# Regrouped attention products and re-placed loads in a fused gated-attention and feed-forward kernel

## The reference

```python
f = 1.0 / (1.0 + np.exp(-f_logit))            # q, k, v, f_logit: 4 x 8 x 768 x 48
for t in range(S):
    state = f[:, :, t, :, None] * state + einsum('bhd,bhe->bhde', k[:, :, t], v[:, :, t])
    y[:, :, t] = einsum('bhd,bhde->bhe', q[:, :, t], state)
x = y as (3072 tokens, 384)
h = x @ w_in;  x = where(h > 0, h, exp(min(h, 0)) - 1) @ w_out       # 384 -> 2048 -> 384
h = x @ w_in2; out = (maximum(h, 0) ** 2) @ w_out2                   # 384 -> 2048 -> 384
```

## Time and profile before

| | |
|---|---|
| median of 3 runs | 978.47 us (978.26 to 981.43) |
| profiled execution | 977.67 us |
| its span | 975.9 us, 27520 instructions |
| busy | PE 953.0 us (98%), PE's weight loads 786.8 (81%), DVE 504.7 (52%), ACT 402.1 (41%), POOL 237.8 (24%) |
| mean granted clock of TensorE | 0.996 |
| DMA | 56.87 MB, mean 58 GB/s |

### The profile page before, as it was taken

How to read it: one execution, slowest core, us unless ns; L and a number is a source line. 1 busy time by engine, 2 the same in 40 slices (tenths; PEclk the granted TensorE clock), 3 DMA queues, 4 the chain that set the end, 5 groups by cost and what they waited for, 6 DMA issues and landing times.

```text
span 975.9 us, 27520 instructions
## 1 busy us (share of the span) xinstructions
PE 953.0 (98%) x11636; PEld 786.8 (81%) x11636; DVE 504.7 (52%) x746; ACT 402.1 (41%) x706; POOL 237.8 (24%) x193
## 2 busy tenths in 40 slices
PE   7799989999999999999999999999999999999998
PEld 6677777888888788888878888888888888888897
DVE  7788576565757657563326663343343343433432
ACT  4555545344535443454444453242332422423322
POOL 3002215363635464454423641000000000000000
PEclk9999999999999999999999999999999999999999
DMA  7461422303130212212003331002020020020100
GB/s 240 152 195 41 127 67 68 99 2 100 36 97 24 79 65 69 65 48 68 1 2 109 97 86 66 1 8 58 1 50 14 0 61 3 7 57 0 19 15 33
DMA packets 72426, 56.87 MB, mean 58 GB/s; under 512 B 37248, under 2 KB 64640, under 8 KB 72320
## 3 DMA queue, kind: packets, MB, share of 16 engines
q1 hardware_dynamic: 69472, 43.87, 16.7%
q10 hardware_dynamic: 2848, 11.44, 3.3%
HBM read 45.84 MB, written 9.44 MB: 57 GB/s over the span
## 4 chain that ended last, share of the span: by engine, by line
PE 94%; DVE 2%; issue 2%; ACT 1%; DMA 1%; SPq 0%; DVEq 0%; ACTq 0%
PE ps L1669 8%; PE ps L1665 8%; PE ps L1664 8%; PE ps L1139 7%; PE ps L1688 7%; PE ps L1684 7%; PE ps L1685 7%; PE ps L1278 6%; PE ps L1301 6%; PE ps L1280 5%; PE ps L1287 5%; PE ps L1303 5%; PE ps L1307 5%; PE ps L1208 2%; PE ps L1156 1%
## 5 line engine op out<-in xcount | busy, mean ns | idle before, releaser
L1609 DVE TENSOR_TENSOR g<-g 128x512 f32<-128x512 f32 x96 | 66.8, 696 | 240.9 <-ACT g L1524 240.3
L1524 ACT ACTIVATE g<-ps 128x512 f32<-128x512 f32 x112 | 67.0, 598 | 276.9 <-PE ps L1669 272.6
L694 POOL TENSOR_TENSOR glo<-g,ghi 128x512 fp32r<-128x512 f32 x65 | 89.7, 1379 | 194.0 <-ACT ghi L519 194.0
L1664 PE MATMUL ps<-xhi,wts 128*128 128x512 f32 x336 | 130.9, 390 | 0.0
L1665 PE MATMUL ps<-xhi,wts 128*128 128x512 f32 x336 | 130.9, 390 | 0.0
L878 DVE SCALAR_TENSOR_TENSOR g<-e,g 128x512 f32<-128x512 f32 x80 | 57.9, 724 | 140.3 <-ACT g L513 140.3
L512 ACT ACTIVATE e<-ps 128x512 f32<-128x512 f32 x80 | 47.9, 598 | 162.6 <-PE ps L1287 162.6
L1684 PE MATMUL ps<-ghi,wts 128*128 128x512 f32 x294 | 114.4, 389 | 0.0
L1685 PE MATMUL ps<-ghi,wts 128*128 128x512 f32 x294 | 114.4, 389 | 0.0
L1278 PE MATMUL ps<-xhi,wts 128*128 128x512 f32 x240 | 98.9, 412 | 0.2 <-ACT g L513 0.2
L1669 PE MATMUL ps<-xlo,wts 128*128 128x512 f32 x336 | 94.6, 390 | 0.0
(11 more groups left out here) (132 smaller groups left out, 1559.4 us busy)
## 6 DMA issues: line engine op xcount, KB each, us to landing
raw<-w SPq DMA_DIRECT2D x52, 192.0 KB, 2.4
q<-qk SPq DMA_DIRECT2D x22, 256.0 KB, 5.0
gate<-fl SPq DMA_DIRECT2D x10, 512.0 KB, 5.5
k<-qk SPq DMA_DIRECT2D x10, 512.0 KB, 3.7
x<-xo ACTq DMA_DIRECT2D x6, 768.0 KB, 3.3
xs<-x ACTq DMA_DIRECT2D x6, 768.0 KB, 4.4
v<-vn SPq DMA_DIRECT2D x11, 384.0 KB, 4.0
krow<-vn SPq DMA_DIRECT2D x20, 192.0 KB, 4.5
```

Source lines behind the costliest of these rows:

```text
L694: nc.gpsimd.tensor_tensor(out=glo[:, f % 2, :], in0=g[:, f % 2, :], in1=ghi[:, f % 2, :].bitcast(F32), op=ALU.subtract).then_inc(s_glo, 1)
L1664: nc.tensor.matmul(h, w(0, k), xhi[:, k, :], start=(k == 0), stop=False)
```

## The change

The steady period of PE has five groups of small products: `product(c, h, 4)` (with `last_column` of the unit before in front of it, from unit 5 on), 5 and 0, 6 and 1, 2 and the transposes, and one of 288: q_state part 0, product 3 of the next unit, q_state part 1, both values and new_state. Slot 15 of a unit moves behind the first group of the next. The last unit keeps six groups. PSUM banks of level 2 change from unit 5 on (`level_pair`), and with them PE's waits. SP, ACT, POOL and DVE are reordered to match; `acc_copy` becomes three copies with a semaphore each. In the start and in the first two periods SP's loads move, DVE's takes of level 1 come before the activation that preceded them, and weight splits move later. The diff, cut to its core:

```diff
...
+        if past(c, h, 5):
+            return pair(c, h, "Y" if l < 2 else "A")
         if past(c, h, 3):
...
         return 2 * c + h + n < UNITS
+
+    def unit_before(c, h):
+
+        return divmod(2 * c + h - 1, 2)
...
         def period(c, h):
-            f = 8 * h
             if more(c, h, 2):
                 load_gates(c, h + 2)
-            if more(c, h, 2):
                 load_k(c, h + 2)
+                load_q(c, h + 2)
             if more(c, h):
+                sp.wait_ge(*level(s_mm, c, h + 1, 4))
                 load_v(c, h + 1)
                 load_staged_v(c, h + 1)
-            if more(c, h, 2):
-                load_q(c, h + 2)
...
             sp.wait_ge(*level(s_mm, 1, 0, 1))
+            load_weights(range(18, 20))
+            load_gates(1, 2)
+            sp.wait_ge(*level(s_mm, 1, 0, 2))
             load_staged_v(1, 0)
-            load_weights(range(18, 20))
-            sp.wait_ge(*level(s_mm, 1, 0, 2))
+            load_weights(range(20, 22))
+            sp.wait_ge(*level(s_mm, 1, 0, 4))
+            load_weights(range(22, 24))
             load_v(1, 0)
-            load_weights(range(20, 22))
-            sp.wait_ge(*level(s_mm, 1, 0, 3))
-            load_gates(1, 2)
-            load_weights(range(22, 24))
             sp.wait_ge(*level(s_mm, 1, 1, 1))
...
             load_k(1, 3)
+            load_q(1, 3)
+            sp.wait_ge(*level(s_mm, 1, 2, 4))
             load_v(1, 2)
             load_staged_v(1, 2)
-            load_q(1, 3)
...
         sp.wait_ge(*level(s_mm, 0, 0, 1))
-        load_weights(range(0, 2))
+        load_gates(1, 1)
+        load_weights(range(1))
         sp.wait_ge(*level(s_mm, 0, 0, 2))
+        load_q(1, 0)
+        sp.wait_ge(*level(s_mm, 0, 1, 1))
+        load_weights(range(1, 2))
         load_staged_v(0, 0)
-        load_gates(1, 1)
-        sp.wait_ge(*level(s_mm, 0, 0, 3))
-        load_weights(range(2, 4))
-        sp.wait_ge(*level(s_mm, 0, 1, 2))
-        load_weights(range(4, 6))
         sp.wait_ge(*level(s_mm, 0, 0, 4))
         load_staged_v(0, 1)
-        load_weights(range(6, 7))
-        sp.wait_ge(*level(s_mm, 0, 1, 3))
-        load_weights(range(7, 9))
+        load_v(0, 0)
         sp.wait_ge(*level(s_mm, 0, 0, 5))
-        load_weights(range(9, 10))
-        load_v(0, 0)
-        sp.wait_ge(*level(s_mm, 0, 1, 4))
-        load_weights(range(10, STAGED))
-        sp.wait_ge(*level(s_mm, 0, 1, 5))
+        load_weights(range(2, 4))
+        sp.wait_ge(*level(s_mm, 0, 0, 6))
         load_v(0, 1)
-        load_q(1, 0)
-        sp.wait_ge(s_kT, 1)
         load_k(1, 0)
+        load_weights(range(4, 6))
+        sp.wait_ge(s_y, 1)
+        load_weights(range(6, STAGED))
         sp.wait_ge(s_last, 1)
...
                 act.wait_ge(s_x2, c * 16 - 32)
-            nc.scalar.activation(xo[:, :, :], ps[:, ACC:ACC + KD, :], ACT.Copy).then_inc(s_acc, 1)
+            for m in range(KD):
+                done = nc.scalar.activation(xo[:, m, :], ps[:, ACC + m, :], ACT.Copy)
+                done.then_inc(s_acc if m == KD - 1 else s_accs, 1)
...
             f = 8 * h
+            if past(c, h, 5):
+                y_copy(*unit_before(c, h))
             hidden_copies(c, f - 1)
...
             hidden_copies(c, f)
+            take5(c, h)
+            high(c, f)
             if h == 0:
                 acc_copy(c)
-            high(c, f)
             hidden_copies(c, f + 1)
-            take5(c, h)
             if h == 0:
...
             high(c, f + 1)
+            pad_v(c, h)
+            take6(c, h)
             hidden_copies(c, f + 2)
             high(c, f + 2)
-            pad_v(c, h)
-            take6(c, h)
             hidden_copies(c, f + 3)
...
             high(c, f + 5)
-            y_copy(c, h)
             hidden_copies(c, f + 6)
+            if not more(c, h):
+                y_copy(c, h)
             high(c, f + 6)
...
         gates(1, 0, True)
-        split_weights(range(0, 2))
         gates(1, 1, True)
+        split_weights(range(0, 1))
         nc.scalar.activation(warm[:, 1:2], warm[:, 0:1], ACT.Exp)
+        split_weights(range(1, 2))
         pad_v(0, 0)
-        split_weights(range(2, 3))
         take4(0, 0)
-        split_weights(range(3, 4))
         take5(0, 0)
...
         take5(0, 1)
+        split_weights(range(2, 4))
         take6(0, 1)
...
             f = 8 * h
+            k_update(c, h, 4)
             low(c, f - 1)
-            k_update(c, h, 4)
             if more(c, h):
                 keep_last(c, h + 1)
+            k_update(c, h, 5)
+            low(c, f)
+            if more(c, h):
                 k_update(c, h + 1, 0)
-            low(c, f)
-            k_update(c, h, 5)
+            low(c, f + 1)
+            k_update(c, h, 6)
             if more(c, h):
                 k_update(c, h + 1, 1)
-            low(c, f + 1)
             low(c, f + 2)
-            k_update(c, h, 6)
+            low(c, f + 3)
             if more(c, h):
                 k_update(c, h + 1, 2)
-            low(c, f + 3)
+            low(c, f + 4)
             if more(c, h):
                 k_update(c, h + 1, 3)
-            low(c, f + 4)
             decay_state(c, h)
...
             f = 8 * h
+            step(c, h, 4)
             activate(c, f - 1)
...
                 x_split(c)
-            if more(c, h):
-                take(c, h + 1, 0)
-            q_update(c, h, 4)
-            take(c, h, 4)
-            if more(c, h):
-                q_update(c, h + 1, 0)
-                double(c, h + 1, 0)
-            double(c, h, 4)
             activate(c, f)
...
             if more(c, h):
-                step(c, h + 1, 1)
+                take(c, h + 1, 0)
+                q_update(c, h + 1, 0)
+                double(c, h + 1, 0)
             activate(c, f + 1)
-            activate(c, f + 2)
             step(c, h, 6)
             if more(c, h):
-                step(c, h + 1, 2)
+                step(c, h + 1, 1)
+            activate(c, f + 2)
             activate(c, f + 3)
...
             if more(c, h):
-                step(c, h + 1, 3)
+                step(c, h + 1, 2)
             activate(c, f + 4)
...
                 reciprocals(c, h + 2, 1)
+            if more(c, h):
+                take(c, h + 1, 3)
+                q_update(c, h + 1, 3)
+                double(c, h + 1, 3)
             state_update(c, h)
...
             low(1, 5)
-            split_weights(split_at(1, 5))
             q_update(1, 0, 5)
             own_updates(1, 1, 1)
+            take(1, 1, 1)
             activate(1, 6)
-            rest(1, 0, 5)
-            rest(1, 1, 1)
+            double(1, 0, 5)
+            double(1, 1, 1)
             low(1, 6)
...
             own_updates(1, 1, 2)
+            split_weights(split_at(1, 5))
             activate(1, 7)
...
             rest(1, 1, 4)
-            rest(1, 2, 0)
-            split_weights(split_at(1, 10))
+            take(1, 2, 0)
             activate(1, 11)
-            low(1, 11)
+            double(1, 2, 0)
             q_update(1, 1, 5)
             own_updates(1, 2, 1)
+            low(1, 11)
+            take(1, 2, 1)
             activate(1, 12)
-            rest(1, 1, 5)
-            rest(1, 2, 1)
+            double(1, 1, 5)
+            double(1, 2, 1)
             low(1, 12)
...
             take(1, 2, 2)
+            split_weights(range(28, 29))
             activate(1, 13)
-            split_weights(split_at(1, 12))
             low(1, 13)
...
             q_update(1, 1, 6)
-            rest(1, 1, 6)
+            double(1, 1, 6)
             step(1, 2, 3)
...
             low(1, 14)
+            split_weights(range(30, 31))
             state_update(1, 1)
+            split_weights(range(29, 32, 2))
...
                     pe.wait_ge(*taken(c, h, l - 1))
-            elif l in (1, 2):
+            elif l == (2 if past(c, h, 5) else 3):
+                pe.wait_ge(s_ev6, count(c, h, 1, 0))
+            elif l in (1, 2, 3):
                 pe.wait_ge(*taken(c, h, l))
-            elif l == 3:
-                pe.wait_ge(s_ev6, count(c, h, 1, 0))
             elif l == 4:
...
             elif more(c, h):
-                pe.wait_ge(*taken(c, h + 1, EARLY - 1))
+                pe.wait_ge(*taken(c, h + 1, 2 if past(c, h, 4) else EARLY - 1))
             else:
...
                 pe.wait_ge(s_krow, count(c, h, 1, 1))
+            elif past(c, h, 4) and more(c, h):
+                pe.wait_ge(*level(s_mm, c, h + 1, 3))
             else:
...
                 pe.wait_ge(s_wlo[1], f + 1 if c == 1 else NF + f + 1)
-            if f == 0 and begun(c, 0, 1):
-                pe.wait_ge(s_acc, c - 1)
             start, stop = n == NF, n == 2 * NF - 1
             for m in range(KD):
+                if f == 0 and begun(c, 0, 1):
+                    pe.wait_ge(*((s_acc, c - 1) if m == KD - 1 else (s_accs, (c - 2) * (KD - 1) + (m + 1))))
                 nc.tensor.matmul(ps[:, ACC + m, :], wts[:, n, 0, m * P:(m + 1) * P], ghi[:, f % 2, :],
...
```

(43 more changed lines are left out.)

## The result

| | before | after |
|---|---|---|
| median of the timed runs | 979.22 us (978.26 to 981.43, 4 runs) | 985.85 us (984.88 to 986.56, 4 runs) |
| ratio of after to before | | 1.0062, 95% interval 1.0044 to 1.0081 |
| profiled execution, its span | 977.67, 975.9 us | 986.56, 984.8 us |

The changed kernel is slower by 6.6 us by the medians and by 8.9 between the two profiled executions. Forecast were 979.2 and "no difference that can be told"; 985.85 lies above the range's end of 984.5.

What follows compares the result with a forecast made beforehand. PE (TensorE) was taken to bound the kernel, 94% of the chain. Terms: -0.8 + 8.75 - 0.5 - 2.7 - 0.7 - 1.2 + 0.4 - 2.5 = +0.75 on 977.67, so 978.4 profiled, 979.2 median; range 972.5 to 984.5.

Steps and rivals of the forecast that it cites:

- Code in the long group: Seven 288-product groups: PE waits for its next instruction block, 1.25 us a period, +8.75 us (3.8 to 10.5).
- the code comes in time: Rival: each instruction block arrives during the one before, the +8.75 falls away, 970.5 us, faster; chance 0.17.
- (d): Stall of 1.35 us before 150.41, at product(2,0,4): stays or grows, +0.4 us (-1.35 to +1.5).
- Moved steps of the steady periods: Reordered copies, takes and loads in the steady periods: forecast 0; x_split at chunk starts priced 0 to 0.5, 4 times.
- Groups: One group's entry and exit saved in 7 steady periods, less added changes of kind: -0.8 us (-1.4 to +1.4).
- The state group's -0.5: The old state group's code stall of 0.54 us, seen once in the steady periods, goes: -0.5 us.
- (a): PE's 2.39 us wait for take(1,2,1) goes as the take comes earlier: -2.4, and 0.3 with `ghi` of step 11.
- (b): PE's 0.70 us wait at 89.83 for take(1,1,1) goes as the take comes earlier: -0.7 us.
- (c): Stall of 1.17 us before 75.67 goes, the gate and weight loads being issued elsewhere: -1.2 (0 if a later block is hit).
- The first 50 us: Later weight loads free DMA queues for PE's stalls at 32 us and before 43.34: -2.5 us (-4.5 to +3).
- the weights come too late: Rival: chunk 6 or 11 lands 3 us late, delaying krow_copy(0,1) or xhi; -2.5 becomes +1 and more, 983; chance 0.08.
- The third rival: q's load in the long group gets ahead of the block's packet: 1.8 us stalls, 12.6 not 8.75, 983.1, slower; chance 0.22.

Runs made afterwards that it cites:

- e3: The changed kernel with output step 11 (nine large products) moved into the long group behind q_state part 1, making groups of 128 and 160; 980.92 us.
- e4: The changed kernel with output step 11 moved into the long group behind the first values, making groups of 192 and 96; 980.85 us.
- e7: The changed kernel with VectorE's x_split ahead of activate(c, f - 1) at the start of a chunk; 983.54 us, measured once.
- e1: The kernel before with only the new start and the new first and second period; 974.23 us against 979.84, ratio 0.994.
- e6: The changed kernel with q's load moved out of the long group, behind v and staged v; 993.11 us, measured once.
- e8: e1 with SP's order of loads in the steady periods as in the changed kernel, other engines in the old six groups; 972.81 us, ratio 0.9931.
- e5: e1 with weights 6 to 11 loaded right behind 4 and 5, not behind the first unit's values; 972.81 us, ratio 0.9934.
- e10: The changed kernel with output step 11 behind q_state part 1, x_split ahead of the first activation, and weights 4 to 11 together; 979.53 us, ratio 1.0006.

## Why the prediction was wrong

The mechanism was the right one; the sum failed in the sizes of its terms. The main term was too small by 2.0 us (8.75 for 10.8), and the last unit (2.0), the end of `product(2,0,4)` (1.7) and VectorE's third split (1.5) were set too low or at nothing, while the first 50 us gave 1.9 less than forecast. No single one of these makes the error. Against the profiled executions, 8.9 us instead of 0.75:

- **Code in the long group: +8.75, measured +10.8.** Places, number and kind were as forecast: seven stalls, 127 products behind a block's beginning. "3.3 - 2.0 = 1.25 us a period" was mis-sized: a block takes 3.37 us, and 127 small products take only 1.83; the difference as written is 1.3 besides, which gives 9.1. The result lies above the term's own upper bound of 10.5. That it is the code is shown by e3 and e4. The rival *the code comes in time* (0.17) fell with the first of these stalls.
- **The last unit: not in the sum, +2.0.** I counted the seven periods with 288 products and took the last unit's order as unchanged. Its y group has 224 in one piece, though, a block begins at product 98, and 127 matmuls on, one large product behind the group's end, PE waits, after's timeline:

```profile
503.09 1.78 PE L1220 MATMUL ps<-PT,vz 64*32 64x128 f32 x128
504.81 0.50 PE L1290 MATMUL ps<-xhi,wts 128*128 128x512 f32 x1
507.02 0.40 PE L1292 MATMUL ps<-xhi,wts 128*128 128x512 f32 x1 [1.71 <-issue]
```

- **(d), product(2,0,4): +0.4, about +2.1.** The stall grew from 1.54 (1.35 in the bracket of the earlier trace rows) to 2.08, within my bounds. Behind it eight large products ran at the lower level of 1.2 GHz, 0.2 us longer each, which the term did not hold; windows of after:

```profile
145.00:148.00 3.00, 3.00 (x10) 2.36 (x10) 0.33 (x2) 0.58 (x2) 0.28 (x1) 0.65 0.89 270
148.00:151.00 3.00, 3.00 (x15) 2.20 (x13) 2.39 (x4) 2.58 (x6) 0.34 (x1) 1.00 0.50 163
```

- **Moved steps of the steady periods: 0, +1.5.** "VectorE's third is about level with its use" was right, and no slack was left for an instruction that takes 1.77 us instead of 0.69. The term's own upper end, 0.5 a chunk, had no row for two engines at once. Shown by e7.
- **Groups: -0.8, about -1.8.** Without stalls and the wait for xlo a steady period takes 45.17 us instead of 45.38, 0.2 us seven times; the other 0.3 are what is left at the two ends of the steady part, where an eighth group is gone (slot 15 of unit (1,1) no longer stands between last_column and `product(2,0,4)`). What the change of kind cost (0 to 0.4 feared) was not measured by itself.
- **The state group's -0.5, and (a), (b), (c), together -4.3 without the 0.3 for `ghi`:** right. The waits of 2.39, 0.70 and 1.17 us are gone, and the stretch gave 5.2 against 4.6 forecast.
- **The first 50 us: -2.5, measured -0.6,** with the scatter of 2.8 us told above, so the size of this miss is not certain. The 2.58 before 43.34 is gone in after and 0.2 in e1; in e3, e4, e6, e7 and e8, whose start is the same, PE waits 0.7 to 1.3 us at the same matmul. Of the stall at 32 us nothing went (before and after, PE's matmul 728 starts at 32.32 and 32.02). krow_copy(0,1) ran at 41.87, close to the 42.4 of the text. Late next were weights 8 to 11, for which ACT waited; ACT's timeline of after, beside the earlier trace rows:

```profile
41.44 0.52 ACT L491 ACTIVATE wts<-stage 128x384 fp32r<-128x384 f32 x1 [1.91 <-DMA stage<-w]
41.87 1.01 ACT L476 ACTIVATE e<-ps 128x1024 f32<-128x1024 f32 x1
42.77 0.51 ACT L491 ACTIVATE wts<-stage 128x384 fp32r<-128x384 f32 x1
45.29 1.99 ACT L491 ACTIVATE wts<-stage 128x384 fp32r<-128x384 f32 x4 [2.00 <-DMA stage<-w]
```

  xhi was ready 1.1 us earlier, not 2, and the first hidden step again ran at half pace. In kind this is the rival *the weights come too late*, at about half its size (1.9 of 3.5 us). The rows show ACT's wait for the weights; that it made the 1.9 us is not shown, since with the weights sooner the start took from 52.80 (e5) to 56.35 us (e10).

The steady part's terms add to 10.8 + 2.0 - 0.5 + 2.1 + 1.5 - 1.8 = 14.1, the 14.1 measured; the 0.3 in the term of the groups is the remainder, so the sum closes by that. The third rival had the sign and nearly the size (983.1), but its reason, q's load, does not carry: e6 takes the load away and keeps 9.0 of the 10.8 us. That its time came near was luck. The 0.22 it got should have gone to "the block takes longer than one quiet example shows": my 3.3 rested on one block out of 85, and the seven of after range from 2.96 to 3.72.

## What to carry to other kernels

On a streamed program, count PE's instructions between large products: where more than one block's worth (here 127 matmuls with their weight loads) of matmuls this small stand in a row, each further block costs a stall of 1 to 2 us, more than the few tenths that one group less saves. Two parts of a change can have opposite signs: here the early part alone was worth 5.6 us and more loads moved brought it to 7.5, while the new steady part cost 14. Compare executions by stretches: e7's profile is 3.1 us shorter than after's, but only 0.9 in the part that the edit touched. When steps are moved so that they are just in time, ask which other engine will then run beside them.

## What the runs showed of the hardware that was not expected

- In the seven long groups of after the block's time has three parts: 0.3 to 1.4 us from its beginning to the start of the next packet, 0.93 to 1.32 for the packet, and 1.3 to 1.6 from the packet's end to the next instruction. With q's load moved away their mean sum fell by only 0.3 us. Where large products stand in the block the first part can be longer: 3.2 us beside a load of gates (e1), 4.8 in e10.
- The clock can make a stall cost twice. Behind the stalls at 143.07 of after and 428.32 of e10, 8 and 12 large products ran at 1.2 GHz. But the stalls of 1.88 at 228.29 and 2.11 at 462.56 in after were followed by a granted clock of 1.00, and the stall at `product(2,0,4)` of 1.54 in before by 1.00, the one of 1.56 in e1 by 0.56. What sets the two kinds apart was not tried.
- VectorE's subtraction of two tiles took 1.77 us instead of 0.69 beside GpSimd's of the same kind (after), and 0.69 again once the two no longer met (e7).
